# Attention with two feed-forward blocks: the last 64 keys of two heads turned and multiplied together, their scores interleaved, loops written out

## The chip, the cores and the metric

One core of one Trainium2 chip runs the whole kernel as one program. The metric is device time in microseconds (us), the median of several executions. The engines are TensorE (PE; its weight loads are listed apart as PEld), VectorE (DVE), ScalarE (ACT), GpSimd (POOL) and SyncE (SP, which here only issues DMAs). Each takes its own instructions in order, and they meet through semaphores.

## The reference

Attention keeps, for each query, only the 32 largest of 576 scores, and two feed-forward blocks follow. There are 2 batches, 8 heads, 576 positions, head size 64.

```python
scores = scale * np.matmul(q, k.transpose(0, 1, 3, 2))
kth = np.partition(scores, -top_k, axis=-1)[..., -top_k:-top_k + 1]
scores = np.where(scores >= kth, scores, -1000000000.0)
attn = np.exp(scores - np.max(scores, axis=-1, keepdims=True))
attn = attn / (np.sum(attn, axis=-1, keepdims=True) + 1e-09)
x = np.matmul(attn, v)                  # heads side by side: 1152 tokens x 512
h = x @ w_in                            # 512 -> 2048
y = (np.maximum(h, 0.0) + alpha * np.minimum(h, 0.0)) @ w_out   # -> 512
out = (y @ w_a * (y @ w_b)) @ w_out2    # 512 -> 1536 -> 512
```

## The kernel before

**Tiles and pairs.** Queries are cut into nine tiles of 128. Tile 0 is the split tile: the last 64 queries of both batches. The others are four whole tiles of batch 0 and four of batch 1. A tile is worked in four pairs of heads, so there are 36 pairs. A pair's two heads lie on partitions 0 to 63 and 64 to 127 of `k_sb` and `q_sb`, so a score matmul uses 64 rows of TensorE's array, and each head has two of the four PSUM banks of `sc_ps`.

**The way of a pair.** TensorE makes the scores (`score`, L777; L772 and L774 for the split tile). ScalarE copies them to `s_sb` (`copy_scores`, L491). VectorE finds the 32 largest of each row (`rank`: four MAX8, L688, and three MATCH_REPLACE8, L698, for each head). GpSimd makes the two bounds (L438, L440), ScalarE a relu that marks what lies below the 32nd value (`relu`, L499), GpSimd subtracts it (L447), ScalarE takes the exponent (`exp`, L505). TensorE turns each head's 576 keys: four 128x128 transposes into `t_ps` (L791) and the last 64 keys into a corner of `o_ps` (L792). ScalarE copies both to `pT` (`evict_turned`, L514 and L515). TensorE multiplies with the values (`times_v`, L806 and L808: five blocks of keys, the fifth of 64, each for queries 0 to 63 and 64 to 127 apart). ScalarE copies four heads at a time to `x_sb` (L576), GpSimd divides by the sums (L428).

**Fp32.** A matmul of fp32 stands in the trace as two MATMULs; the first feed-forward product uses fp32r in a high and a low part (L845, L847, L849).

**Steps.** The program is a list of steps, one for each pair. In the step of pair n TensorE turns and multiplies pair n and makes the scores of pair n+3, VectorE ranks pair n+2, ScalarE and GpSimd mask and exponentiate pair n+1. Between these, TensorE works off the first feed-forward block of the two tiles that came before, cut into four shares per step:

```python
            def step(pair, output, work1=None, n=0):
                if output is not None:
                    turn(output, 0)
                score(pair)
                if work1 is not None:
                    block1(work1, work1.share(n, 0))
                if output is not None:
                    times_v(output, 0)
                    turn(output, 1)
                if work1 is not None:
                    block1(work1, work1.share(n, 1))
                if output is not None:
                    times_v(output, 1)
                if work1 is not None:
                    block1(work1, work1.share(n, 2) + work1.share(n, 3))
```

A share holds items: "turn" (four transposes, L824), "up" (the product into one block of the 2048 hidden columns, 12 MATMULs of L845 to L849; ScalarE's two relus L540 and L541 and GpSimd's L416 and L420 follow) and "down" (L859). `m_ps` has two banks, so an item waits until the last but one is read out.

**Stages.** Six opening steps have no feed-forward work. A section of eight steps follows with the split tile's block (narrow, so few items), and then three sections of eight steps, one for each two tiles; these three are one loop (`Fori`). In this text they are sections 1, 2 and 3, and their steps are 0 to 7: step 0 has the "turn" items, steps 1 to 3 and the start of 4 have "up" items, the rest "down" items. The loop always makes `score(n+3)` and `rank(n+2)`, so that its last steps make scores of three pairs (two of them ranked) that nothing uses. After attention TensorE does the first block of the last two tiles alone, and then the second block (L901 to L916).

**DMAs.** SP issues all of them: queries, keys and values at the start, `w_in` in eight chunks through a two-slot stage (L301), later `w_out` and the other weights. In the loop, keys and values are loaded again in every section.

Of the kernel before, what the change touches and what calls it, by code (L numbers as in the profile page):

```python
# [4 lines left out]
B, H, S, D = 2, 8, 576, 64  # L22
# [29 lines left out]
SECTION = 2 * PAIRS  # L52


def attention_ffn(nc, qT, qT_split, kT, v, w_in, w_out, alpha, w_a, w_b, w_o, out):
# [3 lines left out]
    with ctx:  # L59
# [26 lines left out]
        v_sb, _ = new("v_sb", [P, KC, DM])  # L86
# [4 lines left out]
        pT, _ = new("pT", [P, 2, KC * P])  # L91
# [20 lines left out]
        v1_sb = at("v1_sb", [P, KC, DM], reg_b + 4 * PAIRS * S)  # L112
        qs_sb = at("qs_sb", [P, PAIRS, P], reg_b + 4 * PAIRS * S + 4 * KC * DM)
# [45 lines left out]
        pT_out = sem("pT_out")  # L159
        pv_done = sem("pv_done")  # L160
# [21 lines left out]
        gate = sem("gate")  # L182
        block = ctx.enter_context(nc.Block())

        def started(value):

            return not isinstance(value, int) or value > 0

        def hold(eng, value):

            if not isinstance(value, int):
                eng.sem_inc(gate, 1)

        def attention_loads_landed(eng):

            for p in range(PAIRS):
                eng.wait_ge(k_in[p], 16 * GROUPS)
                eng.wait_ge(v_in[p], 32 * GROUPS)
            for j in range(2):
                eng.wait_ge(q_in[j], 16 * (GROUPS + 1))  # L200

        class Pair:


            def __init__(self, i, split, g):
                before = 0 if split else 1 + 2 * g  # L210
                self.hp, self.split = i % PAIRS, split
                self.j = 1 if split else i // PAIRS
                self.tile = before + i // PAIRS
                self.number = before * PAIRS + i
                self.u = 2 * self.number
                self.halves = 2 * before + i // 2
                self.par, self.ring = i % 2, i % 4

                self.k_loads = g if not (isinstance(g, int) and g == 0) else 1
                self.v_loads = self.q_loads = g + 1  # L220

        def in_groups(g, i):
            return Pair(i, False, g) if i < SECTION else Pair(i - SECTION, False, g + 1)

        def split_pair(i):
            return Pair(i, True, 0)


        OPENING = [split_pair(i) for i in range(PAIRS)] + [Pair(i, False, 0) for i in range(3)]
        OPENING_STEPS = PAIRS + 2  # L230

        def last_of_tile(g):

            if isinstance(g, int) and g == 0:
                return split_pair(PAIRS - 1)
            return Pair(SECTION - 1, False, g - 1)

        class Block1:

# [16 lines left out]


# [11 lines left out]
        def block1_before(g):  # L269

            return Block1([1], SPLIT_AT, 0, 0, 0) if isinstance(g, int) and g == 0 else block1_group(g - 1)
# [26 lines left out]
        def _(sp):  # L298
# [3 lines left out]

            sp.dma_start(qs_sb[:, 0, :], qT_split[:, 0, :]).then_inc(qs_in, 16)
# [8 lines left out]
            for p in range(PAIRS):  # L312
                cols = slice(p * P, p * P + P)
                sp.dma_start(v_sb[:, 0:WHOLE, cols], v[0, 0:WHOLE * P, cols].rearrange("(c p) n -> p c n", p=P))\
                  .then_inc(v_in[p], 16)
                sp.dma_start(v_sb[0:REST, WHOLE, cols], v[0, WHOLE * P:S, cols]).then_inc(v_in[p], 16)
                if p == 0:
                    sp.dma_start(v1_sb[:, 0:WHOLE, :], v[1, 0:WHOLE * P, :].rearrange("(c p) n -> p c n", p=P))\
                      .then_inc(v1_in, 16)
                    sp.dma_start(v1_sb[0:REST, WHOLE, :], v[1, WHOLE * P:S, :]).then_inc(v1_in, 16)  # L320
# [9 lines left out]
            for j in range(2):  # L330

                sp.wait_ge(scored, H * (j + 2))
                sp.dma_start(q_sb[:, j, :, :], qT[2 + j]).then_inc(q_in[j], 16)
            with sp.Fori(1, GROUPS) as g:
                batch = g // 2

                tile = WHOLE + 2 * (g // 2)
                for p in range(PAIRS):

                    sp.wait_ge(pv_done, 2 * H * g + 2 * (p + 1))  # L340
                    hold(sp, g)
                    cols = slice(p * P, p * P + P)
                    sp.dma_start(v_sb[:, 0:WHOLE, cols],
                                 v[bass.ds(batch, 1), 0:WHOLE * P, cols].rearrange("b (c p) n -> p (b c) n", p=P))\
                      .then_inc(v_in[p], 16)
                    sp.dma_start(v_sb[0:REST, WHOLE, cols],
                                 v[bass.ds(batch, 1), WHOLE * P:S, cols].rearrange("b p n -> p (b n)"))\
                      .then_inc(v_in[p], 16)

                sp.wait_ge(scored, 2 * H * g + 2 * H)  # L350
                hold(sp, g)
                sp.dma_start(q_sb[:, 0, :, :], qT[bass.ds(tile, 1)].rearrange("t p a q -> p (t a) q"))\
                  .then_inc(q_in[0], 16)
                for p in range(PAIRS):
# [25 lines left out]
            with sp.Fori(1, PASSES2) as t:  # L380
                second_pass(t)
# [589 lines left out]
```

## Time and profile before

| | us |
|---|---|
| median of 3 runs | 713.56 (712.17 to 714.42) |
| span of the profiled execution | 711.5 |
| TensorE busy in it | 659.2 (93%) |
| VectorE busy | 446.4 (63%) |
| ScalarE busy | 346.1 (49%) |
| GpSimd busy | 253.6 (36%) |

The span runs from the first to the last instruction; the median of the runs is 2.06 us longer. The profiled execution has no separate time beside its span here, so the difference to the median is carried over. In the slices of the page TensorE is at 4 to 8 tenths in the first fifth and at 9 in nearly all of the rest; VectorE is at 9 or more in the first fifth.

### The profile page before, as it was taken

To read this page: it belongs to the slowest core of one execution; us is meant where nothing else is said; L and a number is where in the kernel's file an instruction comes from. 1 tells how busy PE (TensorE), PEld (TensorE's weight loads), DVE (VectorE), ACT (ScalarE), POOL (GpSimd) and SP (SyncE) were. 2 spreads that over 40 slices of the span, in tenths; PEclk is the share of its full clock that TensorE was granted. 3 is DMA by queue.
4 is the path that set the end of the run, shared out by engine and by line. 5 is a ranking of instruction groups with operands and counts; after the bars stand their busy time and mean duration, and the time that the engine had idled before them with its cause. 6 is when DMAs were issued, how large, how long until landed. Compare 5 with 4: busy or idle time off the path is not lost.

```text
span 711.5 us, 13571 instructions
## 1 busy us (share of the span) xinstructions
PE 659.2 (93%) x4904; PEld 568.7 (80%) x4904; DVE 446.4 (63%) x895; ACT 346.1 (49%) x788; POOL 253.6 (36%) x349
## 2 busy tenths in 40 slices
PE   4578789989999999999999989999999999999997
PEld 2245577768887788887888879989999999999996
DVE  5999999999988799888898732433222211121112
ACT  3666666668664587645776544533212311131112
POOL 2666566257752477613777227600000000000000
PEclk9986999999999999999999999999999999999999
DMA  8522401111110110111102002451100100010001
GB/s 306 151 90 93 160 2 33 34 35 34 44 35 24 34 35 18 50 34 34 35 18 77 1 1 68 132 171 60 60 0 1 45 1 0 1 44 0 0 0 44
DMA packets 23591, 35.67 MB, mean 50 GB/s; under 512 B 1840, under 2 KB 11312, under 8 KB 23536
## 3 DMA queue, kind: packets, MB, share of 16 engines
q1 hardware_dynamic: 23536, 34.88, 15.4%
q8 instruction: 41, 0.67, 0.4%
q14 instruction: 14, 0.11, 0.0%
HBM read 32.51 MB, written 2.36 MB: 49 GB/s over the span
## 4 chain that ended last, share of the span: by engine, by line
PE 63%; DVE 22%; issue 8%; POOL 4%; ACT 2%; DMA 0%; POOLq 0%; ACTq 0%; SPq 0%; DVEq 0%
PE m_ps L859 12%; DVE top L688 12%; DVE work L698 9%; PE sc_ps L903 7%; PE sc_ps L901 7%; PE sc_ps L902 7%; PE m_ps L845 4%; PE o_ps L806 3%; PE m_ps L847 3%; PE m_ps L849 3%; PE sc_ps L777 3%; PE t_ps L791 2%; POOL p_sb L447 2%; PE t_ps L915 1%; PE o_ps L916 1%
## 5 line engine op out<-in xcount | busy, mean ns | idle before, releaser
L688 DVE MAX8 top<-work 128x8 f32<-128x576 f32 x228 | 160.6, 746 | 0.0
L447 POOL TENSOR_TENSOR p_sb<-s_sb,p_sb 128x576 f32<-128x576 f32 x74 | 104.0, 1415 | 86.8 <-ACT p_sb L499 86.8
L859 PE MATMUL m_ps<-g_sb,wout 128*128 128x256 f32 (+1 forms) x640 | 134.4, 363 | 0.0
L859 PEld LDWEIGHTS m_ps<-g_sb,wout 128*128 128x128 f32 x640 | 109.7, 190 | 17.4 <-issue 4.6
L736 DVE TENSOR_TENSOR ab<-sc_ps,a_sb 128x384 f32<-128x384 f32 x36 | 20.1, 557 | 146.9 <-PE sc_ps L903 146.9
L698 DVE MATCH_REPLACE8 work<-top,work 128x576 f32<-128x576 f32 x152 | 111.8, 743 | 0.0
L806 PE MATMUL o_ps<-v_sb,pT 128*64 128x64 f32 (+1 forms) x720 | 71.8, 239 | 20.5 <-ACT pT L515 20.5
L806 PEld LDWEIGHTS o_ps<-v_sb,pT 128*64 128x64 f32 (+1 forms) x720 | 55.9, 144 | 43.5 <-issue 35.2
L845 PE MATMUL m_ps<-xT_parts,win_hi 128*128 128x256 f32 x256 | 76.6, 299 | 2.9 <-issue 2.9
L688 DVE MAX8 top<-s_sb 128x8 f32<-128x576 f32 x76 | 55.0, 749 | 37.0 <-ACT s_sb L491 37.0
L847 PE MATMUL m_ps<-xT_parts,win_hi 128*128 128x256 f32 x256 | 73.0, 285 | 0.0
L849 PE MATMUL m_ps<-xT_parts,win_lo 128*128 128x256 f32 x256 | 72.9, 285 | 0.0
L808 PE MATMUL o_ps<-v_sb,pT 128*64 128x64 f32 (+1 forms) x720 | 71.8, 240 | 0.0
L499 ACT ACTIVATE p_sb<-s_sb,kth_big 128x576 f32<-128x576 f32 x74 | 53.2, 768 | 29.2 <-POOL neg_max L440 29.2
L514 ACT ACTIVATE pT<-t_ps 128x512 f32<-128x512 f32 x72 | 42.8, 594 | 47.6 <-PE o_ps L792 47.6
L491 ACT ACTIVATE s_sb<-sc_ps 128x576 f32<-128x576 f32 x78 | 50.3, 646 | 26.0 <-POOL p_sb L447 17.9
L633 ACT ACTIVATE a_sb<-sc_ps 128x384 f32<-128x384 f32 x36 | 17.7, 492 | 92.0 <-PE sc_ps L903 91.9
L420 POOL TENSOR_TENSOR g_sb<-pos_neg 128x256 f32<-128x256 f32 (+1 forms) x80 | 58.5, 731 | 6.7
L791 PE MATMUL t_ps<-ident,p_sb 128*128 128x128 f32 x288 | 49.0, 296 | 9.8 <-ACT p_sb L505 4.8
L638 ACT ACTIVATE ab_hi<-ab 128x384 fp32r<-128x384 f32 x36 | 18.9, 525 | 78.5 <-DVE ab L736 78.5
L505 ACT ACTIVATE p_sb<-p_sb,neg_max 128x576 f32<-128x576 f32 x74 | 56.9, 769 | 0.0
L845 PEld LDWEIGHTS m_ps<-xT_parts,win_hi 128*128 128x128 f32 x256 | 49.4, 193 | 9.0 <-issue 7.8
(90 smaller groups left out, 1429.3 us busy)
## 6 DMA issues: line engine op xcount, KB each, us to landing
k_sb<-in_kT SPq DMA_DIRECT2D x20, 288.0 KB, 3.3
stage<-in_w_in SPq DMA_DIRECT2D x8, 512.0 KB, 4.6
v_sb<-in_v SPq DMA_DIRECT2D x16, 256.0 KB, 2.8
wout<-in_w_out SPq DMA_DIRECT2D x1, 4096.0 KB, 14.9
stage<-in_w_a SPq DMA_DIRECT2D x8, 384.0 KB, 3.1
stage<-in_w_b SPq DMA_DIRECT2D x8, 384.0 KB, 3.1
stage<-in_w_o SPq DMA_DIRECT2D x6, 512.0 KB, 3.4
q_sb<-in_qT SPq DMA_DIRECT2D x10, 256.0 KB, 3.3
```

The costliest lines, as they stand in the source:

```text
L420: nc.gpsimd.tensor_tensor(g_sb[:, f, 0:n], pos[:, f % 2, 0:n], neg[:, f % 2, 0:n], ALU.add).then_inc(g_done, 1)
L447: nc.gpsimd.tensor_tensor(p_sb[:, row, :], s_sb[:, row, :], p_sb[:, row, :], ALU.subtract).then_inc(masked, 1)
L505: nc.scalar.activation(p_sb[:, row, :], p_sb[:, row, :], ACT.Exp, bias=neg_max[:, pair.ring, c:c + 1], scale=SCALE, accum_out=sums[:, pair ...
L688: largest = nc.vector.max(top32[:, row, 8 * r:8 * r + 8], work[:, c, :] if r else s_sb[:, row, :])
L698: nc.vector.match_replace(work[:, c, :], top32[:, row, 8 * r:8 * r + 8], work[:, c, :] if r else s_sb[:, row, :], -3.0e38)\
L791: nc.tensor.transpose(t_ps[:, k * P:(k + 1) * P], p_sb[:, row, k * P:(k + 1) * P], ident[:, :])
L806: nc.tensor.matmul(o_ps[0:REST, dst], pT[0:rows, c, k * P:k * P + REST], v_sb[0:rows, k, cols], start=(k == 0), stop=(k == KC - 1))
L808: done = nc.tensor.matmul(o_ps[REST:P, dst], pT[0:rows, c, k * P + REST:(k + 1) * P], (v1_sb if pair.split else v_sb)[0:rows, k, cols], st ...
L845: nc.tensor.matmul(m_ps[:, bank, 0:n], win_hi[:, k, cols], xT_hi[:, k, 0:n], start=(k == 0), stop=False)
L847: nc.tensor.matmul(m_ps[:, bank, 0:n], win_hi[:, k, cols], xT_lo[:, k, 0:n], start=False, stop=False)
L849: done = nc.tensor.matmul(m_ps[:, bank, 0:n], win_lo[:, k, cols], xT_hi[:, k, 0:n], start=False, stop=(k == DC - 1))
L859: done = nc.tensor.matmul(m_ps[:, bank, 0:n], wout[:, f, d * P:(d + 1) * P], g_sb[:, f, 0:n], start=(f == 0), stop=(f == FC1 - 1))
```

## The change

Keys of the second head of each pair are rotated by 64 on the host, so that its last 64 keys come first and lie in memory right behind the first head's last 64. Both are then one 128x128 transpose (`both`), copied to a new buffer `pR`. Their values lie in `vr_sb`, 128 rows of 128 columns for each pair, with zeros where one head's keys meet the other head's columns (VectorE writes them once, DMAs write the rest). `times_v` is now one call for both heads: eight blocks of 128 keys, then one product for the last keys of both, 128 columns wide. It stands where the second head's product stood. `score` alternates the heads and waits once for both heads' copies. All loops are written out; scores and ranks of pairs that don't exist are not made; batch 1's keys and values are loaded once. Each value load of a pair is three DMAs instead of two.

```diff
-        v_sb, _ = new("v_sb", [P, KC, DM])
+        v_sb, _ = new("v_sb", [P, WHOLE, DM])
+        vr_sb, _ = new("vr_sb", [P, PAIRS, P])
-        pT, _ = new("pT", [P, 2, KC * P])
+        pT, _ = new("pT", [P, 2, WHOLE * P])
+        pR, _ = new("pR", [P, P])
...
+        def pair(number):
+            return Pair(number) if 0 <= number < N_PAIRS else None
...
+            def load_v(batch, p):
+                cols = slice(p * P, p * P + P)
+                sp.dma_start(v_sb[:, :, cols], v[batch, 0:WHOLE * P, cols].rearrange("(c p) n -> p c n", p=P))\
+                  .then_inc(v_in[p], 16)
+                for c in range(2):
+                    sp.dma_start(vr_sb[c * D:(c + 1) * D, p, c * D:(c + 1) * D],
+                                 v[batch, WHOLE * P:S, p * P + c * D:p * P + (c + 1) * D]).then_inc(v_in[p], 16)
...
             def evict_turned(pair, c):
 
                 act.wait_ge(turned, pair.u + c + 1)
-                if started(pair.u + c - 1):
-                    act.wait_ge(pv_done, pair.u + c - 1)
-                nc.scalar.activation(pT[:, c, 0:WHOLE * P], t_ps[:, :], ACT.Copy)
-                nc.scalar.activation(pT[0:REST, c, WHOLE * P:KC * P], o_ps[0:REST, 4 * D:4 * D + P],
-                                     ACT.Copy).then_inc(pT_out, 1)
+                if c == 0 and pair.number:
+
+                    act.wait_ge(pv_done, pair.u)
+                nc.scalar.activation(pT[:, c, :], t_ps[:, :], ACT.Copy).then_inc(pT_out, 1)
+                if c:
+                    nc.scalar.activation(pR[:, :], o_ps[:, 4 * D:4 * D + P], ACT.Copy).then_inc(rest_out, 1)
...
+                if pair.number:
+
+                    pe.wait_ge(copied, pair.u)
+                for x in range(2):
+                    cols = slice(x * HALF, (x + 1) * HALF)
+                    for c in range(2):
+                        rows = slice(c * D, (c + 1) * D)
...
                 for k in range(WHOLE):
-                    nc.tensor.transpose(t_ps[:, k * P:(k + 1) * P], p_sb[:, row, k * P:(k + 1) * P], ident[:, :])
-                nc.tensor.transpose(o_ps[0:REST, 4 * D:4 * D + P], p_sb[:, row, WHOLE * P:S], ident[:, :])\
-                  .then_inc(turned, 1)
...
+                if c:
+                    if pair.hp % 2 == 0 and pair.halves:
+
+                        pe.wait_ge(o_out, pair.halves)
+                    both = p_sb[:, row - 1:row + 1, :].rearrange("p c n -> p (c n)")
+                    done = nc.tensor.transpose(o_ps[:, 4 * D:4 * D + P], both[:, WHOLE * P:WHOLE * P + P], ident[:, :])
+                done.then_inc(turned, 1)
...
                 if work1 is not None:
                     block1(work1, work1.share(n, 0))
                 if output is not None:
-                    times_v(output, 0)
                     turn(output, 1)
                 if work1 is not None:
                     block1(work1, work1.share(n, 1))
                 if output is not None:
-                    times_v(output, 1)
+                    times_v(output)
```

What stands on TensorE in an "up" step of a later section (step 2), before; the rows left out repeat the up items' or the value products' lines:

```order
L777 MATMUL sc_ps<-k_sb,q_sb 128x288 [waits copied]
...
L845 MATMUL m_ps<-xT_parts,win_hi 128x256 [waits m_free]
...
L806 MATMUL o_ps<-v_sb,pT 64x64 [waits pT_out,v_in2]
L808 MATMUL o_ps<-v_sb,pT 64x64
...
L791 MATMUL t_ps<-ident,p_sb 128x128 [waits pT_out,expd]
L791 MATMUL t_ps<-ident,p_sb 128x128 x3
L792 MATMUL o_ps<-ident,p_sb 64x128
...
L819 REGISTER_ALU
```

The same place in the changed program, whose line numbers are its own:

```order
L688 MATMUL sc_ps<-k_sb,q_sb 128x288 x3
L770 MATMUL m_ps<-xT_parts,win_hi 128x256 [waits m_free]
...
L702 MATMUL t_ps<-ident,p_sb 128x128 [waits pT_out,expd]
L702 MATMUL t_ps<-ident,p_sb 128x128 x3
L708 MATMUL o_ps<-ident,p_sb 128x128
...
L728 MATMUL o_ps<-v_sb,pT 64x64 [waits rest_out,pT_out,v_in3]
L730 MATMUL o_ps<-v_sb,pT 64x64
...
L733 MATMUL o_ps<-vr_sb,pR 64x128
L735 MATMUL o_ps<-vr_sb,pR 64x128
```

The first head's product no longer stands ahead of the second head's transposes. It has moved behind them and behind the share that follows, to where TensorE waits for the copies of both heads. Register instructions (L819) are gone.

On SP, in the opening, the value loads of the first pair and of batch 1 (for the split tile) stood so before:

```order
L314 DMA v_sb<-in_v 128x4x128
L316 DMA v_sb<-in_v 64x128
L318 DMA v_sb<-in_v 128x4x512
L320 DMA v_sb<-in_v 64x512
L321 DMA alpha_sb<-in_alpha 128x16
```

and in the changed program:

```order
L259 DMA v_sb<-in_v 128x4x128
L262 DMA vr_sb<-in_v 64x64 x2
L277 DMA v_sb<-in_v 128x4x512
L280 DMA vr_sb<-in_v 64x4x64 x2
L283 DMA alpha_sb<-in_alpha 128x16
```

Five more DMAs (one for each of the four pairs, one for batch 1) now stand ahead of the third chunk of `w_in`.

## Rows read from the trace of the kernel before

**Rows 1.** The page: span, and busy time (share) and instructions by engine
```profile
span 711.5 us, 13571 instructions
PE 659.2 (93%) x4904; PEld 568.7 (80%) x4904; DVE 446.4 (63%) x895; ACT 346.1 (49%) x788; POOL 253.6 (36%) x349
```

**Rows 2.** Windows: stretch, length, busy of PE, PEld, DVE, ACT, POOL, clock, DMA
```profile
85.00:155.00 70.00, 60.38 (x626) 50.72 (x628) 68.77 (x150) 46.17 (x118) 35.64 (x60) 0.98 0.09 26
248.60:339.80 91.20, 89.48 (x793) 74.31 (x792) 78.17 (x162) 58.13 (x140) 49.51 (x71) 1.00 0.12 33
```

**Rows 3.** Waits of PE from 150 us on: total us, times, longest
```profile
PE m_ps L824 <- POOL x_sb L428: 3.2, 3, 1.8
PE o_ps L806 <- ACT pT L515: 2.4, 7, 0.5
```

**Rows 4.** PE timeline, scores of one pair; the first row: window 215.38 to 215.42
```profile
215.39 0.52 PE L777 MATMUL sc_ps<-k_sb,q_sb 64*128 64x288 f32 x2
...
215.19 0.27 PE L792 MATMUL o_ps<-ident,p_sb 128*64 128x128 f32 x1
215.39 1.25 PE L777 MATMUL sc_ps<-k_sb,q_sb 64*128 64x288 f32 x8
216.57 0.48 PE L859 MATMUL m_ps<-g_sb,wout 128*128 128x256 f32 x1
```

**Rows 5.** Group of L859 by shape, then PE timeline: values of one head
```profile
L859 PE MATMUL m_ps<-g_sb,wout 128*128 128x256 f32 x512 | 117.8, 383 | 0.0
...
209.80 0.59 PE L859 MATMUL m_ps<-g_sb,wout 128*128 128x256 f32 x2
210.32 0.27 PE L806 MATMUL o_ps<-v_sb,pT 128*64 128x64 f32 x1
210.43 0.22 PE L806 MATMUL o_ps<-v_sb,pT 128*64 128x64 f32 x1
...
210.78 0.22 PE L806 MATMUL o_ps<-v_sb,pT 128*64 128x64 f32 x1
...
210.94 0.27 PE L806 MATMUL o_ps<-v_sb,pT 64*64 64x64 f32 x1
...
211.20 0.70 PE L859 MATMUL m_ps<-g_sb,wout 128*128 128x256 f32 x2
```

**Rows 6.** Timeline, step 2 of section 3; in brackets idle time and its releaser
```profile
350.59 0.60 PE L791 MATMUL t_ps<-ident,p_sb 128*128 128x128 f32 x4
350.87 0.38 ACT L540 ACTIVATE pos_neg<-m_ps 128x256 f32<-128x256 f32 x1 [0.50 <-PE m_ps L849]
...
351.74 0.48 POOL L416 TENSOR_SCALAR pos_neg<-pos_neg,alpha_sb 128x256 f32<-128x256 f32 x1 [0.15 <-ACT pos_neg L541]
...
353.13 0.19 POOL L438 TENSOR_SCALAR kth_big<-top 128x2 f32<-128x2 f32 x1
...
353.61 1.44 ACT L499 ACTIVATE p_sb<-s_sb,kth_big 128x576 f32<-128x576 f32 x2 [1.44 <-POOL neg_max L440]
...
356.94 0.27 ACT L515 ACTIVATE pT<-o_ps 64x128 f32<-64x128 f32 x1
...
357.35 0.24 PE L806 MATMUL o_ps<-v_sb,pT 128*64 128x64 f32 x1 [0.25 <-ACT pT L515]
```

**Rows 7.** Timeline, a "down" step of section 2: second head's copy and product
```profile
313.17 0.60 ACT L514 ACTIVATE pT<-t_ps 128x512 f32<-128x512 f32 x1 [0.49 <-PE o_ps L792]
...
314.79 0.27 PE L806 MATMUL o_ps<-v_sb,pT 128*64 128x64 f32 x1
```

**Rows 8.** Timeline of the opening: SP's issue, ScalarE's copy, VectorE's next rank
```profile
8.29 0.58 SPq L316 DMA_DIRECT2D v_sb<-in_v  x1
...
25.34 0.63 ACT L491 ACTIVATE s_sb<-sc_ps 128x576 f32<-128x576 f32 x1
...
27.48 1.41 DVE L688 MAX8 top<-s_sb 128x8 f32<-128x576 f32 x2
```

**Rows 9.** Windows: the five us in which the granted clock had fallen
```profile
155.00:160.00 5.00, 5.00 (x38) 3.75 (x35) 5.00 (x10) 3.20 (x9) 3.05 (x4) 0.66 0.02 5
```

More of the change, by code:

```diff
@@ L181, in attention_ffn, with __init__ @@
         stored = sem("stored")
-        gate = sem("gate")
         block = ctx.enter_context(nc.Block())
[L185 to L200, printed above, removed]
-        class Pair:
[L209 to L236, printed above, removed]
+        class Pair:
+            def __init__(self, number):
+                self.number, self.u = number, 2 * number
+                self.tile, self.hp = divmod(number, PAIRS)
+                self.split = self.tile == 0
+                self.j = 1 if self.split else (self.tile - 1) % 2
+                self.batch = 0 if self.split else (self.tile - 1) // WHOLE
+                self.halves = 2 * self.tile + self.hp // 2
+                self.par, self.ring = number % 2, number % 4
+        def pair(number):
+            return Pair(number) if 0 <= number < N_PAIRS else None
         class Block1:
@@ L629, in second_pass @@
             def second_pass(t):
-                first = not started(t)
+                first = t == 0
                 for f in range(FC2):
@@ L652, in _ @@
                 hi_of_w2(c)
-            second_pass(0)
-            with act.Fori(1, PASSES2) as t:
+            for t in range(PASSES2):
                 second_pass(t)
@@ L673, in add_h, with rank @@
                                                 mybir.AxisListType.X, ALU.add).then_inc(m_free, 1)
-            def rank(pair, n, output=None, split_block1=None):
+            def rank(pair, output, split_block1, n):
                 rounds = TOPK // 8
                 for r in range(rounds):
-                    for c in range(2):
+                    for c in range(2 if pair is not None else 0):
                         row = 2 * pair.par + c
@@ L693, in rank @@
                             largest.then_inc(ranked, 1)
-                    for c in range(2 if r < rounds - 1 else 0):
+                    for c in range(2 if pair is not None and r < rounds - 1 else 0):
                         row = 2 * pair.par + c
-                        dve.wait_ge(rank_step, 12 * n + 4 * r + c + 1)
+                        dve.wait_ge(rank_step, 12 * pair.number + 4 * r + c + 1)
                         nc.vector.match_replace(work[:, c, :], top32[:, row, 8 * r:8 * r + 8],
@@ L749, in _ @@
                     lo_of_y(0, 0)
-            second_pass(0)
-            with dve.Fori(1, PASSES2) as t:
+            for t in range(PASSES2):
                 second_pass(t)
@@ L816, in block1 @@
                     use, bank = work1.use(item)
-                    if started(use - 1) and (item[0] != "down" or item[2] == 0):
+                    if use > 1 and (item[0] != "down" or item[2] == 0):
                         pe.wait_ge(m_free, use - 1)
@@ L936, in second_pass @@
                 times_w_o(t, FC2 - 1)
-            second_pass(0)
-            with pe.Fori(1, PASSES2) as t:
+            for t in range(PASSES2):
                 second_pass(t)
```

260 lines of the change are left out of this document (113 added, 147 removed).

## The prediction

> **What bounds the kernel now.** I read the page first, then windows along the span, then the waits of TensorE, then the timeline of single steps. The page gives a span of 711.5 us with TensorE busy for 659.2 [rows 1]; the reader should see that one engine is busy for 93%, but not yet that it is the bound everywhere. The windows cut this in two. From 85 to 155 us VectorE is busy 68.77 of 70 us and TensorE 60.38 [rows 2]: the ranks are the bound there, as from about 8 us on, and faster TensorE work before roughly 157 us buys nothing. From 248.6 to 339.8 us (section 2) TensorE is busy 89.48 of 91.2 and VectorE 78.17 [rows 2]; from 150 us to the end TensorE's named waits come to a few us [rows 3]. There TensorE is the bound, so the change can earn in the 24 steps of sections 1 to 3. What follows (feed-forward alone) it doesn't touch.
>
> One thing the busy share hides. In section 3's step 2 TensorE starts its second `times_v` at 357.35, 0.25 us after it had nothing to do, released by ScalarE's copy, which ended at 356.94 + 0.27 = 357.21 [rows 6]. That copy is the end of a chain with no slack: the last up item of the step before, ScalarE's relus from 350.87, GpSimd from 351.74 with the bounds behind them in its queue (353.13), ScalarE's relu for the mask from 353.61 (it sat idle 1.44 us for it), GpSimd's mask, the next score copy, then the transposed scores' copy [rows 6]. The step begins at 350.59, so the copies are ready 6.62 us later, however early TensorE comes.
>
> **Part by part. Scores interleaved: nothing.** The code before issues head 0's four MATMULs and then head 1's. A window of 0.04 us holds two of them at once, 0.52 us together [rows 4], and all eight take 1.25 us, 0.4 to 0.5 us each: four rounds of two. The halves of the array already work side by side, so alternating them in the program changes neither the rounds nor the end. If it helped at all, the bound is half of the 1.18 us from 215.39 to 216.57 [rows 4], 0.59 for a pair. I take zero, by the nearest row.
>
> By the Trainium skill, "TensorE: Matmul & The Clock Gate", Part 3, "The mechanism", matmuls start and end strictly in program order and only weight loads are pulled ahead. By that rule the order before would not overlap the heads and the interleaving would be worth up to the bound just named; the two simultaneous starts speak against it.
>
> **Transposes.** Four of L791 take 0.60 us from the start of the first to the end of the last, and in rows 4 the next begins 0.20 us ahead of the scores; starts lie about 0.11 us apart (0.60 less one's 0.27, by three). A pair has nine instead of ten: 0.11 saved.
>
> **Values.** One head between two down matmuls before: the row of two at 209.80 ends at 210.39, and one takes 0.38, so the second starts at 210.01 and the usual distance is 0.21 to 0.22. Then 0.31 to the first L806, 0.88 from 210.32 to 211.20, and 0.32 to the second matmul behind (211.20 + 0.70 - 0.38) [rows 5]. Less two usual distances that is 1.07. Where a transpose follows instead it is 1.03 at most, so two heads cost 2.1. The 0.88 holds: 0.11 for the first, six distances of 0.058 (210.43 to 210.78), 0.16 to 210.94 where the tile shape changes from 128*64 to 64*64, and 0.26 for the last keys [rows 5]. Now both heads in one go: 0.88, plus eight more starts at 0.058 (0.47), less the 0.10 of the change of shape and 0.05 of a slow first start, plus 0.12 because the last product is 128 columns wide, twice 0.058: 1.32. With the 0.31 and 0.32 around it, less 0.43, it is 1.5. Saved: 2.1 - 1.5 = 0.6, with the transpose **0.7 us a step** where TensorE is not made to wait.
>
> **Where it waits.** "Down" steps: ScalarE had waited 0.49 us for the transposes, started the copy at 313.17, and TensorE came for it only at 314.79 [rows 7]: about 0.9 us of slack. The change brings transposes and product forward by the same amount, so the slack stays. Steps 4 to 7 gain: 4 x 0.7 = 2.8 us a section. Steps 2 and 3: the copies are ready at +6.62 as before. The first head's product used to be done ahead of this wait and now stands behind it, so what follows starts 1.32 - 0.88 = 0.44 later. TensorE idles some 1.4 us (0.25 plus 1.03 plus 0.11) and the step gets longer by 0.44. Against that, register instructions between waits are gone; GpSimd's 0.15 us of idle ahead of L416 [rows 6] is the most one hop of that chain can give back. I take 0.1, so 0.3 lost, twice: -0.6. Steps 0 and 1: step 0 waits for GpSimd's division (3.2 us in three sections [rows 3]), one small copy less on ScalarE (at most its 0.27) and one transpose less bring that forward; step 1 gains its own, together 0.7. A section saves 2.8 - 0.6 + 0.7 = 2.9, three sections 8.7. In section 1 the first two steps still stand behind VectorE's backlog, -0.7: **8.0**.
>
> **Pairs that don't exist.** 36 instead of 39 scores, the three in steps 5 to 7 of section 3, on the bound. One costs 215.19 to 216.57 = 1.38 [rows 4] (less a usual 0.11, plus a slow first weight load of 0.11): 3 x 1.38 = **4.1**. The ranks and masks that go with them run beside TensorE: nothing.
>
> **The opening.** Five more DMAs at about 0.58 us an issue [rows 8] put the third `w_in` chunk up to 2.9 us later. ScalarE converts it ahead of the copy at 25.34, which VectorE needs for the second MAX8 after 27.48, at 28.1 [rows 8]: 28.1 - 25.97 = 2.1 us of cover. The queue is full there anyway, so I take less than that: 0. Both ends: 0 to 0.8, and 3.7 if each DMA took twice the row. VectorE's zero fill stands ahead of its first rank, when it has nothing else; it costs the memset's time if the first scores were early. Loops written out, keys and values loaded once: no wait on them in the rows of the waits, so 0; the waits now merged (both heads' copies before any score) fall in step 1 only, where the second head's half ended the stretch before too.
>
> **Sum:** 8.0 + 4.1 = 12.1. Against the profiled span: 711.5 - 12.1 = 699.4; the median lies 2.06 above its span, so **701.4**. Its own range is 697 to 705: 0.2 us either way in each of 20 steps.
>
> **The rivals.** (A) The chain in steps 1 to 3 moves with TensorE, since it begins at TensorE's last item, and something in it shortens: all 24 steps gain 0.7, 16.8 + 4.1 = 20.9, 692.6. For it: VectorE has 13 us of air in a section. Against it: the wait of 0.25 us is there already. (B) The heads' scores did not overlap before and do now: 0.59 x 21 pairs under the bound = 12.4 more, 689.0; against it the two starts of rows 4. It is also what the skill's page (named above) would have. (C) The opening loses the 3.7 us: 705.1, up to 708 if later chunks lose too. (D) Slower: the granted clock. Around 155 us, behind a TensorE wait of 1.8 us for L428 [rows 3] amid transposes, the mean clock over five us was 0.66 [rows 9], so at 1.2 instead of 2.4 GHz for part of it; 0.34 x 5 = 1.7 us lost if TensorE is the bound. The change makes waits of 1.4 to 1.5 us in steps 0, 2 and 3 of each section, nine in all. If every one brings a fall: 15.3, 716.7. It decides from the seventh fall on (7 x 1.7 = 11.9). Against it: the waits are shorter than the 1.8 and two thirds stand amid dense up items. (E) The gain in steps 4 to 7 is eaten by VectorE or by ScalarE's order (in them scores are copied only once a mask is done), and only the dropped scores remain: 709.4. That is also how it looks if the change does not do what it says in the steps: 3 of 39 score blocks gone and nothing else.
>
> **Numbers.** Forecast 0.60; A 0.12; B 0.02; C 0.09; D 0.07; E 0.10. The range 692 to 708 holds forecast, A and C and leaves out 0.19. About 0.3% (2.1 us) is what a measurement here can tell from no change, so 711.4 is the border. Half of E I count as within it: faster 0.60 + 0.12 + 0.02 + 0.09 + 0.05 = 0.88, same 0.05, slower 0.07.
>
> **What the changed profile would show.** Right: steps 4 to 7 shorter by 0.7 and steps 2 and 3 longer by 0.3, with some 1.4 us of TensorE's wait on the new `pR` copy in each; scores of a pair still 1.25 us; the value block 1.3 us from first to last start of the next matmul, without a gap at the last keys; section 2 near 88.3 us; section 1 beginning near 157 us as before. Wrong: TensorE's wait spread over steps 4 to 7 (E), a start of section 1 after 158 us (C), clock below 0.97 in sections 2 and 3 (D), scores near 0.7 us (B). A missing wait in steps 2 and 3 would mean A. The weakest link is the claim that the chain of rows 6 repeats unmoved when TensorE's order changes around it.

## The result, and the profile after

The changed kernel takes 702.9 us (median of 4 runs, 702.61 to 704.17), the kernel before beside it 713.29 (712.17 to 714.42). The ratio is 0.9862, with a 95% interval of 0.9845 to 0.9879: faster by 10.4 us, where 701.4 had been forecast. The page of the changed kernel answers to [rows 1]:

```profile
span 700.8 us, 11978 instructions
PE 624.0 (89%) x4700; PEld 549.9 (78%) x4700; DVE 428.0 (61%) x859; ACT 334.2 (48%) x740; POOL 250.4 (36%) x345
```

TensorE is busy 35.2 us less, but the span is only 10.7 us shorter: part of the saving lies ahead of 157 us, where VectorE is the bound, and part has turned into idle time. The waits of TensorE from 150 us to 420 us, to be held against [rows 3]:

```profile
PE o_ps L728 <- ACT pR L446: 9.7, 7, 1.6
PE m_ps L749 <- POOL x_sb L367: 4.9, 3, 1.6
PE m_ps L770 <- issue: 3.1, 1, 3.1
PE sc_ps L688 <- ACT s_sb L420: 2.5, 3, 0.8
```

The wait for the transposed scores' copy has grown from 2.4 to 9.7 us in seven places, that for GpSimd's division from 3.2 to 4.9, and step 1 of each section now waits 0.8 us for both heads' scores to be copied (the last row). The 3.1 us of L770 stand behind attention, ahead of the first up item of the feed-forward work alone; there were 2.9 before. Windows of sections 2 and 3 and of the start of the feed-forward work alone, first after, then before (the columns are those of [rows 2]):

```profile
240.15:328.12 87.97, 82.61 (x754) 70.52 (x752) 78.03 (x163) 56.68 (x132) 49.58 (x70) 1.00 0.05 16
328.12:411.97 83.85, 78.50 (x730) 68.37 (x729) 52.15 (x109) 50.85 (x120) 47.05 (x65) 1.00 0.00 1
415.00:422.00 7.00, 5.65 (x26) 5.68 (x27) 0.00 (x0) 0.82 (x3) 2.45 (x4) 0.51 0.01 2
```

```profile
241.57:332.83 91.26, 89.54 (x793) 74.34 (x793) 78.16 (x163) 58.12 (x141) 49.57 (x70) 1.00 0.12 33
332.83:423.69 90.86, 89.39 (x793) 74.49 (x793) 71.50 (x149) 58.07 (x140) 50.20 (x69) 1.00 0.10 29
428.50:432.00 3.50, 3.50 (x19) 3.50 (x18) 0.00 (x0) 0.66 (x2) 0.61 (x2) 0.52 0.00 0
```

The first column is the stretch, so its length is the section's: 91.26 to 87.97 and 90.86 to 83.85. In section 2 TensorE is busy 6.93 us less and idle 5.36 in place of 1.72 (length less busy). The last rows hold the stretches in which the clock stood at half, 1.2 instead of 2.4 GHz: 6.8 us after (from 415.2), 3.4 before (from 428.6).

The lengths of section 2's steps, each from its first transpose to that of the next:

| step | 0 | 1 | 2 | 3 | 4 | 5 | 6 | 7 | sum |
|---|---|---|---|---|---|---|---|---|---|
| before | 6.30 | 11.46 | 12.05 | 10.85 | 12.31 | 11.48 | 13.21 | 13.60 | 91.26 |
| after | 6.39 | 10.67 | 12.39 | 11.18 | 11.60 | 10.76 | 12.49 | 12.49 | 87.97 |

In section 3 the last three steps are 9.39, 11.12 and 11.12 after, 1.37 shorter each: the scores that aren't made. Before, step 7 of section 3 took 13.21: the 0.39 more in section 2 is the loop's end. Section 1 has the same steps after, but for step 1 (11.61) and step 2, which takes 12.65 us, 0.60 more than before and not 0.34.

**Where the 10.7 us of the span come from.** Up to section 1 VectorE is the bound, so there the starts of its rank of the same pair are compared. Its eighth pair starts 0.21 us earlier than before, its tenth to 18th 0.52 to 0.59 later: 0.75 lost in the split tile's section. Section 2 starts 1.42 us earlier (240.15 against 241.57), so section 1 gained 1.96; section 2 gained 3.29, section 3 7.01. Behind the last step 1.02 is lost. -0.21 + 0.75 - 1.96 - 3.29 - 7.01 + 1.02 = -10.70.

TensorE's timeline of a "down" step shows the product with both heads' values; in step 2 of section 3 it waits for it:

```profile
310.25 0.59 PE L784 MATMUL m_ps<-g_sb,wout 128*128 128x256 f32 x2
310.77 0.27 PE L728 MATMUL o_ps<-v_sb,pT 128*64 128x64 f32 x1
310.78 0.27 PE L730 MATMUL o_ps<-v_sb,pT 128*64 128x64 f32 x1
...
311.75 0.28 PE L733 MATMUL o_ps<-vr_sb,pR 128*64 128x128 f32 x1
...
312.07 0.70 PE L784 MATMUL m_ps<-g_sb,wout 128*128 128x256 f32 x2
...
345.18 0.60 PE L702 MATMUL t_ps<-ident,p_sb 128*128 128x128 f32 x4
345.71 1.24 PE L688 MATMUL sc_ps<-k_sb,q_sb 64*128 64x288 f32 x8
...
351.85 0.24 PE L728 MATMUL o_ps<-v_sb,pT 128*64 128x64 f32 x1 [1.30 <-ACT pR L446]
```

The block takes 312.07 - 310.77 = 1.30 us, with no change of shape inside it and no gap at the last keys (311.75). The scores still take 1.24. In the up step the product starts 351.85 - 345.18 = 6.67 us into the step; before it was 357.35 - 350.59 = 6.76 [rows 6]. The wait ends with this chain on ScalarE:

```profile
345.38 0.38 ACT L470 ACTIVATE pos_neg<-m_ps 128x256 f32<-128x256 f32 x1 [0.51 <-PE m_ps L774]
...
348.00 1.44 ACT L428 ACTIVATE p_sb<-s_sb,kth_big 128x576 f32<-128x576 f32 x2 [1.47 <-POOL neg_max L377]
349.35 0.36 ACT L470 ACTIVATE pos_neg<-m_ps 128x256 f32<-128x256 f32 x1
...
350.39 0.65 ACT L420 ACTIVATE s_sb<-sc_ps 128x576 f32<-128x576 f32 x1 [0.41 <-POOL p_sb L384]
350.94 0.59 ACT L444 ACTIVATE pT<-t_ps 128x512 f32<-128x512 f32 x1
351.42 0.28 ACT L446 ACTIVATE pR<-o_ps 128x128 f32<-128x128 f32 x1
```

It is the chain of [rows 6] with nearly the same pauses: 1.47 us for GpSimd's bounds (1.44 before) and 0.41 for its mask (0.33 before).

### The profile page after: what moved, and what is told of

It is laid out like the page before. It is cut to its first block, busy times and chain, and to the rows that moved or that the text cites. A ratio compares the mean times of both kernels' runs of the same rounds, so it can differ in the third digit from the quotient of the medians.

```text
span 700.8 us, 11978 instructions
## 1 busy us (share of the span) xinstructions
PE 624.0 (89%) x4700; PEld 549.9 (78%) x4700; DVE 428.0 (61%) x859; ACT 334.2 (48%) x740; POOL 250.4 (36%) x345
## 4 chain that ended last, share of the span: by engine, by line
PE 63%; DVE 21%; POOL 5%; issue 5%; ACT 4%; DMA 0%; SPq 0%; ACTq 0%; POOLq 0%; DVEq 0%
PE m_ps L784 12%; DVE top L607 12%; DVE work L617 9%; PE sc_ps L820 7%; PE sc_ps L818 7%; PE sc_ps L819 7%; PE m_ps L770 4%; PE m_ps L774 3%; PE m_ps L772 3%; POOL p_sb L384 2%; PE o_ps L728 2%; PE sc_ps L688 2%; PE t_ps L702 1%; PE t_ps L832 1%; PE o_ps L833 1%
## 5 line engine op out<-in xcount | busy, mean ns | idle before, releaser
L607 DVE MAX8 top<-work 128x8 f32<-128x576 f32 x216 | 155.0, 773 | 0.0
L384 POOL TENSOR_TENSOR p_sb<-s_sb,p_sb 128x576 f32<-128x576 f32 x72 | 101.3, 1417 | 73.3 <-ACT p_sb L428 73.3
L617 DVE MATCH_REPLACE8 work<-top,work 128x576 f32<-128x576 f32 x144 | 107.9, 772 | 0.0
L728 PE MATMUL o_ps<-v_sb,pT 128*64 128x64 f32 x576 | 45.4, 239 | 40.7 <-ACT pR L446 40.5
L770 PE MATMUL m_ps<-xT_parts,win_hi 128*128 128x256 f32 x256 | 77.1, 301 | 3.1 <-issue 3.1
L728 PEld LDWEIGHTS o_ps<-v_sb,pT 128*64 128x64 f32 x576 | 40.7, 151 | 48.4 <-issue 48.0
L607 DVE MAX8 top<-s_sb 128x8 f32<-128x576 f32 x72 | 52.7, 775 | 25.2 <-ACT s_sb L420 25.2
L420 ACT ACTIVATE s_sb<-sc_ps 128x576 f32<-128x576 f32 x72 | 46.9, 652 | 28.1 <-POOL p_sb L384 20.1
L770 PEld LDWEIGHTS m_ps<-xT_parts,win_hi 128*128 128x128 f32 x256 | 49.9, 195 | 10.1 <-issue 7.9
L617 DVE MATCH_REPLACE8 work<-top,s_sb 128x576 f32<-128x576 f32 x72 | 53.9, 771 | 0.0
L702 PE MATMUL t_ps<-ident,p_sb 128*128 128x128 f32 x288 | 46.9, 288 | 4.9 <-ACT p_sb L434 4.9
```

The source lines that it names most:

```text
L384: nc.gpsimd.tensor_tensor(p_sb[:, row, :], s_sb[:, row, :], p_sb[:, row, :], ALU.subtract).then_inc(masked, 1)
L607: largest = nc.vector.max(top32[:, row, 8 * r:8 * r + 8], work[:, c, :] if r else s_sb[:, row, :])
L617: nc.vector.match_replace(work[:, c, :], top32[:, row, 8 * r:8 * r + 8], work[:, c, :] if r else s_sb[:, row, :], -3.0e38)\
L702: done = nc.tensor.transpose(t_ps[:, k * P:(k + 1) * P], p_sb[:, row, at_key:at_key + P], ident[:, :])
L728: nc.tensor.matmul(o_ps[0:REST, dst], pT[:, c, k * P:k * P + REST], v_sb[:, k, cols], start=first, stop=False, skip_group_check=True)
L770: nc.tensor.matmul(m_ps[:, bank, 0:n], win_hi[:, k, cols], xT_hi[:, k, 0:n], start=(k == 0), stop=False)
```

## The experiments

Ten kernels in three groups (numbers 1 to 4, 5 to 8, 9); each group shared its runs of the kernel before. "Ratio" is to that kernel, with the 95% interval.

**1. The heads' scores in turn, all else as changed.**

```diff
-                for x in range(2):
-                    cols = slice(x * HALF, (x + 1) * HALF)
-                    for c in range(2):
-                        rows = slice(c * D, (c + 1) * D)
+                for c in range(2):
+                    rows = slice(c * D, (c + 1) * D)
+                    for x in range(2):
+                        cols = slice(x * HALF, (x + 1) * HALF)
```

> The changed kernel with its scores in the old order, all of head 0 and then all of head 1. My account (the halves of the array overlapped already): no change, 702.9 within 1 us, and a pair's eight score matmuls still span 1.25 us. Rival (program order rules, and the interleaving brought what the change gained): 0.59 us for each of 21 pairs under the bound come back, 712 to 715, and the eight span near 2 us.

Measured: 703.8 us (702.97 to 703.92), ratio 0.9853 (0.9838 to 0.9867); the changed kernel's 0.9862 lies inside. Section 2 takes 88.05 us (241.05 to 329.10), no step in it more than 0.03 us off the table above. A pair's scores in this kernel:

```profile
241.58 1.25 PE L688 MATMUL sc_ps<-k_sb,q_sb 64*128 64x288 f32 x8
```

Interleaving is worth nothing; the two heads' matmuls run two at a time in either order.

**2. Three blocks of scores put back.** In the last three steps TensorE makes a pair's scores again, from keys and queries that are there; nobody reads them.

```diff
                 if score_of is not None:
                     score(score_of)
+                elif output is not None:
+                    spare_score(output.hp - 1)
```

> The changed kernel with three more score blocks on TensorE alone, in the last three steps of attention, where the kernel before made them; nobody reads them. My account (TensorE is the bound there and a block costs 1.38): 702.9 + 4.1 = 707.0. Rival (what dropping the spare pairs brought came from VectorE, ScalarE and GpSimd, or nothing did): 702.9 to 703.5.

Measured: 706.67 us (706.49 to 707.29), ratio 0.9899 (0.9885 to 0.9913). Steps 5 to 7 of section 3 are 10.76, 12.49 and 12.49 again, as in section 2: 3 x 1.37 = 4.1 us, all on the path. The medians differ by 3.8 from the changed kernel and by 2.9 from number 1 of the same group. Between the profiles of number 1 and of this one, section 3 is 4.1 us longer, and the part behind attention 1.1 us shorter: the clock stood at half there for 6.8 us in number 1 and for 3.4 here.

**3. Only the loops and the pairs that don't exist.** The kernel before, with loops written out, no scores or ranks of absent pairs, batch 1's keys and values loaded once. Heads, transposes and products are those of before.

```diff
-            with pe.Fori(1, GROUPS) as g:
-                section(g)
+            for i in range(FIRST_STEP, N_PAIRS):
+                step(pair(i + 3), pair(i), *block1_at(i))
```

> The kernel before with its loops written out, the spare pairs dropped and batch 1's keys and values loaded once; scores, transposes, copies and value products as before. My account: the dropped scores give 4.1 and the lost register instructions at most 0.15 in each of steps 1 to 3, so 713.3 - 4.1 - 0.6 = 708.6. Rival (written-out loops are worth more than that): under 706, with steps 4 to 7 of sections 1 and 2 shorter too.

Measured: 707.34 us (706.0 to 708.71, with the kernel before at 713.93), ratio 0.9907 (0.9892 to 0.9922). That is 6.6 us, of 10.4 in the whole change; 4.7 had been expected. Section 3's last three steps are 10.10, 11.83 and 11.83 (from 11.48, 13.21, 13.21: 3 x 1.38). In section 2 step 2 takes 11.91 (12.05 before) and step 7 13.21 (13.60); the rest stands, with step 3 at 10.98 there and at 10.71 in the other two sections (10.85 before). So the loop's end costs 0.39 twice, and something that went with the loops costs 0.14 in each of steps 2 and 3. I put it down to the registers, but the repeated loads went too, and no run separates them. TensorE's part after attention is 286.2 us here with no stretch at half clock, 287.8 before with 3.4 us of it: 1.6 us that are not the edit's. The 7.3 us between the two profiles are, to 0.1, these 1.6, the 4.1 of the scores, 0.8 of the loops' ends and 6 x 0.14.

**4. That kernel with the first head's product moved behind the second head's transposes**, both waiting for both copies. This is the placement of the change with the work of before.

```diff
-                pe.wait_ge(pT_out, pair.u + c + 1)
+                pe.wait_ge(pT_out, pair.u + 2)
...
-                    times_v(output, 0)
                     turn(output, 1)
...
                 if output is not None:
+                    times_v(output, 0)
                     times_v(output, 1)
```

> The kernel before with its loops written out and the spare pairs dropped, and both heads' value products (in their old form, five blocks each) behind the second share, where both copies are waited for. Compare with e7, which has them in their old places. My account (in steps 2 and 3 of a section the copies come at a set time after the step's start): each of those six steps gets 0.9 to 1.0 longer, and each of the twelve steps 4 to 7 some 0.15 shorter because the array changes shape less often: e7 + 4, about 713. Rival (the chain to the copies moves with TensorE): only the savings, e7 - 3.6, about 705.

Measured: 717.01 us (716.15 to 721.93), ratio 1.006 (1.0036 to 1.0084), 9.7 us slower than number 3, where 4 had been expected. Steps 4 to 7 are 0.15 shorter each, steps 2 and 3 12.80 and 11.61 to 11.89, that is 0.9 longer. TensorE's waits from 150 us on:

```profile
PE o_ps L704 <- ACT pT L435: 8.9, 8, 1.7
PE m_ps L722 <- POOL x_sb L357: 5.3, 3, 1.8
```

The first row is the new wait (1.9 us in number 3). In sum the placement alone costs time, and it is the joining of the last keys that pays: against number 4 the changed kernel's down steps are 0.56 shorter each. More was lost than steps 2 and 3 explain. Of the 10.4 us between the two profiles, 4.1 come ahead of section 1 (it begins at 152.53 against 148.45), 4.8 in the three sections and 1.5 behind attention, where this profile has 3.4 us at half clock and number 3 none. Step 0 takes 7.59, 8.53 and 7.10 us in place of 7.65, 6.25 and 6.25; in sections 2 and 3 step 1 gives 1.15 and 0.74 of that back. VectorE waits 3.9 us for the split tile's items (1.3 in number 3), and 3.2 of it while TensorE's clock is at half, from 94.1 to 100.9. Which part of the loss is due to the clock, half for 3.4 us from 158.9 and from 251.1 as well, stays open.

**5. The third share ahead of the product, everywhere.** In numbers 5 to 9 the diff is this one, with another condition for `early`; the work is the same.

```diff
+                early = work1 is not None
                 if work1 is not None:
-                    block1(work1, work1.share(n, 1))
+                    block1(work1, work1.share(n, 1) + (work1.share(n, 2) if early else []))
                 if output is not None:
                     times_v(output)
                 if work1 is not None:
-                    block1(work1, work1.share(n, 2) + work1.share(n, 3))
+                    block1(work1, ([] if early else work1.share(n, 2)) + work1.share(n, 3))
```

> The changed kernel with one move on TensorE: in every step the third share of feed-forward items stands ahead of the product with the values instead of behind it. Nothing is left out or added. Theory (the 1.4 us that TensorE idles in steps 2 and 3 of each section is uncovered time of a chain that begins at the step's first items, not a limit on the work): one item of about 1.8 us fills it, six waits of some 1.4 us go, less some 0.5 us each that ScalarE's order gives back because the mask behind the item comes later: -5.4, about 697.5 us, waits of L728 on L446 from 150 us on near nothing, steps 2 and 3 near 10.9 and 10.1 us. If TensorE's items in the split section are also what VectorE waits for, that section gives back another 0.7. Rival (the wait is only moved: the copies come later by as much as the item takes, or m_ps's two banks block the item): 702.9 us, the same total wait in other rows. Slower is possible in steps 4 to 7, where no wait is there to fill: 0.

Measured: 701.73 us (698.88 to 702.29), ratio 0.9822 (0.9801 to 0.9842). Only 1.3 us below the changed kernel of the same group (number 8), where 5.4 had been expected. Section 2's steps 1 to 4 are 10.53, 12.35, 9.58 and 13.61, where they had been 10.67, 12.39, 11.18 and 11.60. Step 3 gains 1.6, step 2 next to nothing, and step 4, the one with the last up and the first down items, loses 2.0.

**6. The same in the split section alone** (`early` where `work1.split`).

> The same move, but only in the eight steps of the split tile's block (from 66 to 151 us in the changed kernel). VectorE adds the halves there and waits for TensorE's items. Theory (both heads' product, now one stretch ahead of the third share, makes these items late, and that costs the 0.5 to 0.8 us by which VectorE falls back between its 8th and 10th pair): section 1 begins 0.7 us earlier, near 150.3, the time is 702.2 us and VectorE's wait for the split block's items falls from 1.6 us to 1.2 or less. Rival (the loss comes from the two falls of the granted clock there and not from the order): 702.9 us, section 1 begins at 151.0 as in the changed kernel. Second rival (VectorE is the bound in this section by its own work and makes up any loss before 157 us): 702.9 as well, but with the wait gone.

Measured: 700.77 us (698.76 to 702.1), ratio 0.9808 (0.9792 to 0.9825), 2.2 below number 8, and section 1 begins at 148.78: more than the 0.7 that had been expected. VectorE's waits from 66 to 151 us, here and then in number 8:

```profile
DVE pos_neg L591 <- PE m_ps L765: 0.5, 1, 0.5
```

```profile
DVE pos_neg L591 <- PE m_ps L765: 3.1, 4, 1.1
```

In the changed kernel's first profile the same row has 1.6, before 1.2. VectorE's 17th pair starts 0.72 us ahead of the kernel before here, 0.53 behind it in the changed kernel's profile and 2.66 in number 8's. Part of the lead goes again in section 1, whose step 1 takes 13.95 us in this profile (11.61 in the changed kernel's): the clock was at half for 3.4 us from 164.9.

**7. The same in steps 2 and 3 of sections 1 to 3 alone.**

> The same move in steps 2 and 3 of sections 1 to 3 alone, six steps in all. Theory (the whole worth of the move lies in the waits of these steps): as much as the move everywhere less what the split section gives, -4.9, about 698.0 us; steps 2 and 3 of section 3 near 11.5 and 10.3 us against 12.39 and 11.16, all other steps as in the changed kernel. Rival (the chain from ScalarE's relus through GpSimd's mask to the copies is the bound of these steps, and the idle time only comes up at the next use of the copies' results): 702.9, with the wait in the following step's scores or transposes.

Measured: 699.63 us (697.58 to 700.52), ratio 0.9798 (0.978 to 0.9817), 3.4 below number 8. Steps 2, 3 and 4 are 12.33, 9.58 and 12.19: 34.10 in place of 35.17, and 3 x 1.07 = 3.2. The expectation had 4.9, with 0.9 from each of steps 2 and 3. In step 2 TensorE waits all the same, but for a bank:

```profile
351.06 0.39 PE L770 MATMUL m_ps<-xT_parts,win_hi 128*128 128x256 f32 x1 [1.06 <-ACT pos_neg L471]
```

The moved item can't start, since ScalarE's relus of an earlier item, which free its bank, stand in ScalarE's queue behind the scores' mask, copies and exponent.

**8. The changed kernel again**, as the measure for numbers 5 to 7.

> The changed kernel itself, once more, so that the small differences of the other three are read against it on the same chip. Expected: 702.9 us, within 0.2%. In its trace: if the granted clock's fall of 6.8 us behind the last attention step (3.4 us in the kernel before) is a matter of the execution, it may be 3.4 or none here, with the part after attention 1.2 to 1.7 us shorter for each 3.4; if it belongs to the changed program, it is 6.8 again. VectorE's MAX8 rows near 745 ns if their 773 ns in the first profile belong to that execution, 773 if to the program.

Measured: 703.0 us (702.5 to 703.86), ratio 0.9846 (0.9833 to 0.986). Section 2's and section 3's steps repeat to 0.04 us. The clock behind attention was at half for 3.4 us:

```profile
414.20:418.00 3.80, 1.22 (x9) 0.74 (x7) 0.00 (x0) 2.45 (x5) 2.04 (x2) 1.00 0.00 0
418.00:421.40 3.40, 2.85 (x13) 2.88 (x14) 0.00 (x0) 0.00 (x0) 0.45 (x1) 0.50 0.02 5
421.40:425.00 3.60, 3.60 (x32) 3.60 (x31) 0.63 (x1) 2.67 (x7) 2.44 (x4) 1.00 0.00 0
```

From the last turn items to the end it took 287.90 us, 288.85 in the first profile with twice that stretch. The longer fall belongs to the execution.

**9. Numbers 6 and 7 together, and then without step 2.**

> The changed kernel with the third share ahead of the values in the split section and in steps 2 and 3 of sections 1 to 3: the two moves that each gained, together. Theory (they act on different stretches, the first on VectorE's lead ahead of section 1, the second on TensorE's waits in it, and add up): against the changed kernel -2.2 and -3.4, 697.4 us from 703.0. Section 2's step 3 near 9.58 and step 4 near 12.19 us as with the second move alone. Rival (TensorE waits for VectorE's divided sums or for the scores' copies in section 1 anyway, so that only one of the two leads can be used): 699.6, as the better of the two alone, with a longer step 1 in section 1 (13.95 us was seen with the first move alone).

> The same without the move in step 2. Theory (in step 2 the moved item waits 1.1 us for a bank of m_ps, since ScalarE's relus of the item before it stand in its queue behind the relu for the mask; step 2 only fell from 12.39 to 12.33 us with the move, so it is worth nothing): the same time as with step 2 moved too, within 0.3 us, and in step 2 TensorE's wait of 1.4 us on the copy of the last keys is back in place of the wait for the bank. Rival (step 2's item being early is what lets step 3 start its own on time): step 3 near 10.5 us in place of 9.58 in each section, 2.7 us slower than with both steps moved.

Measured: with both steps 696.66 us (695.72 to 697.58), ratio 0.9771 (0.9747 to 0.9794): the fastest kernel of the study, 6.3 us below number 8. The kernel before was 0.6 us faster beside this group too (713.25 against 713.85), so 5.7 us is the fairer figure. TensorE's waits from 146.5 to 407 us:

```profile
PE m_ps L749 <- POOL x_sb L367: 6.5, 3, 3.2
PE m_ps L770 <- ACT pos_neg L471: 4.0, 6, 1.3
PE sc_ps L688 <- ACT s_sb L420: 1.7, 2, 0.8
PE o_ps L728 <- ACT pR L446: 1.3, 1, 1.3
```

The wait for the last keys' copy is gone but for one place; a wait for a bank of 4.0 us has come for part of it. The two gains add up: 2.2 + 3.4 = 5.6 expected, 5.7 found. VectorE has no wait for the split tile's items at all, and section 1 begins at 146.49, 4.5 us ahead of the changed kernel. Of that lead 1.4 us go again before section 2, since step 0 takes 9.29 us in place of 6.40: TensorE waits 3.2 us for GpSimd's division, and the clock is at half from 152.8 to 156.2. Without step 2 it is 698.04 us (697.52 to 701.21), ratio 0.9794 (0.977 to 0.9818), the steps 12.39, 9.77 and 12.28, in sum 0.3 us a section longer. The intervals overlap, so step 2's part, 0.9 by the steps, is not told from nothing by the times. Its order in the split section is the same, and yet VectorE waits 1.7 us there, in one place (up to 100.1 us), with the clock at half from 93.2 to 100.0.

## Why the prediction was right

**The bound.** TensorE from 157 us on: right. Three dropped score blocks were worth their full 4.1 (number 2).

**Scores interleaved, 0:** right, shown by number 1. Two starts within 0.04 us in [rows 4] had been enough to say so. The rule of the Trainium skill ("TensorE: Matmul & The Clock Gate", Part 3, "The mechanism") that matmuls start and end in program order would have made the order of the heads matter by up to 0.59 us a pair; the trace differs from it, with 1.24 us for the eight interleaved and 1.25 for head after head.

**Down steps, -0.7 each:** -0.71, -0.72, -0.72 in steps 4 to 6. The value block, worked out as 1.32 from distances of before, is 1.30. Against number 3, which has only the loops and the absent pairs changed, it is the same 0.71 to 0.72. Number 4 splits it: 0.15 comes with the new place of the first head's product, 0.56 with the joined last keys.

**Steps 2 and 3, +0.3 each:** +0.34 and +0.33 in section 2. Both terms can be seen apart: number 3, with the loops written out, is 0.14 shorter there (0.1 had been taken), and from it to the changed kernel it is +0.48 and, where step 3 stood at 10.71, +0.45 (0.44 had been worked out). The claim called the weakest link, that the chain repeats unmoved, held to 0.09 us in step 2 of section 3. In section 1's step 2 it did not hold as well: the product starts 6.93 us into the step, 0.17 later than before, and the step is 0.60 longer.

**Steps 0 and 1, -0.7 together:** +0.09 and -0.79, right as a sum, in part by luck. The division does release TensorE earlier, 4.53 us into the step in place of 4.84 (section 2: 244.68 - 240.15 and 246.41 - 241.57). But the first head's product, once ahead of this wait, now stands behind it, as in steps 2 and 3. So TensorE waits 1.63 us in place of 0.74, and the step gets no shorter. The prediction had worked out this cost for steps 2 and 3 only.

**Mis-sized.** Three terms. First, "loops written out: 0" left out the loop's end, 0.39 us in each of sections 1 and 2, 0.8 in all (number 3). Second, section 1: 2.2 of the 8.0 us were to come from it, 1.96 came, and with the loop's end taken out 1.6. The 157 us named for its start was where TensorE becomes the bound; the section's first transposes stand at 148.38 before and 150.98 after. Third, the sum had no term for the split section and none for what follows attention. The first lost 0.75 us. In it VectorE waits for TensorE's items, and both heads' product, a longer block now, stands ahead of them. Here are its longest such wait in the changed kernel and the window of the 3.4 us before its end (columns of [rows 2]):

```profile
97.92 0.42 DVE L591 TENSOR_REDUCE pos_neg<-m_ps 128x128 f32<-128x256 f32 x1 [1.28 <-PE m_ps L765]
...
94.40:97.80 3.40, 3.40 (x17) 3.40 (x17) 1.89 (x6) 1.31 (x5) 0.83 (x2) 0.51 0.02 5
```

TensorE ran at half clock in that window, and between 70 and 151 us it did so for three stretches of 3.4 us after and for one before. So order and clock are both at work, and the runs separate them only in part. From the start of its 8th pair to that of its 11th VectorE needs 34.6 us before and 34.7 in number 3 (old order). In the five profiles with the changed kernel's order in this section (the changed kernel, numbers 8, 1, 2 and 7) it needs 35.4, 36.8, 36.1, 35.9 and 34.9. In the four with the third share ahead (numbers 5, 6 and both of 9) it needs 33.9, 33.9, 33.3 and 35.1. That the order of TensorE's items counts is shown where the clock agrees: six of these profiles have a stretch of 3.4 us at half clock from between 93 and 94.5 us, and in them VectorE's 10th pair starts 11.9 us after the 9th with the share ahead (numbers 5 and 6) and 12.9 to 13.1 with the changed order (the changed kernel, numbers 8, 1 and 2). That the change itself lost 0.75 by its order is not shown: number 7 has the changed order there and lost 0.3, and the changed kernel lost 0.75 in one execution and 2.2 in the other. The 1.02 at the end is the longer stretch at half clock (number 8: half as long there, 0.95 us less).

In sum: +12.1 forecast, 0.8 more for the loops' ends, 0.6 less in section 1, 0.75 and 1.0 less in the two stretches left out, and 0.2 more in the opening: 10.7, 1.4 less than forecast. The last three are of the size by which executions of the changed kernel differ among themselves (its 8th pair starts 0.2 us earlier than before in one profile, 0.5 later in the other), so how near the forecast came is partly luck; the terms for the steps and for the dropped scores are not.

**The rivals.** A (no wait in steps 2 and 3): no, there are waits of 1.3 us and more. B (the heads' scores overlap only now): no, by number 1. C (opening): no, VectorE's first eight pairs are 0.1 to 0.2 us earlier, and 0.5 later in number 8's profile, far from 3.7. D (falls of the clock from the new waits): none inside sections 1 to 3 of the changed kernel, and the windows of sections 2 and 3 show 1.00. In numbers 6 and 9 there is one fall each in section 1 (from 164.9, 152.8 and 154.7 us), and number 6's step 1 is 2.3 us longer with it: where such a fall comes, it costs. E (the gain in steps 4 to 7 is eaten): no, they gain in full.

**What the expectation of number 5 got wrong:** an idle time of 1.4 us is not a hole of that size. In step 2 what was put into it ran into a bank that the same chain frees, and in step 4 the move delayed what had been on time.

## What to carry to other kernels

When two small pieces are joined into one, price the joined block and the place where it must now stand apart: here joining earned 0.56 us a step and the later place another 0.15, but the later place cost 0.9 in those steps where a chain of other engines delivers the input, and an item moved ahead gave some of it back. Before filling a wait with work, look at which buffer that work needs and who frees it; if it is freed by the chain that is waited for, the wait only changes its name. And where another engine is the bound, look for what it waits for behind a block that gets longer. Last, compare a loss of less than 1 us with what the same program loses from one execution to the next before giving it a cause.

## What the runs showed of the hardware

- Two products on column halves with their own weights start 0.01 us apart (310.77 and 310.78), and 32 of them start within 0.98 us (310.77 to 311.75), 0.06 us for two. The two 64-row halves run side by side even when the program gives one head's matmuls after the other's: eight in 1.25 us in number 1, 1.24 interleaved.
- The recorded duration of VectorE's MAX8 differs between executions of the same program: 773 ns in the changed kernel's first profile, 746 in the second, while the usual distance from pair to pair in the opening is 9.62 or 9.63 us in the first and 9.64 in the second. It is a matter of the record, not of the time. The first profile, then the second:

```profile
L607 DVE MAX8 top<-work 128x8 f32<-128x576 f32 x216 | 155.0, 773 | 0.0
```

```profile
L607 DVE MAX8 top<-work 128x8 f32<-128x576 f32 x216 | 152.1, 746 | 0.0
```

- The stretch at half clock behind attention has another length from execution to execution, 6.8 and 3.4 us for the changed kernel. From the last "turn" items to the end it took 286.2 us without one (number 3), 287.7 to 288.1 with 3.4 us (seven profiles) and 288.9 to 289.4 with 6.8 us (four): 1.5 to 1.9 us for the first stretch, 0.8 to 1.7 for the second.
